# Attention on one core: products with V and row sums in four 32-column tiles instead of two 64-column tiles

## What is computed

```python
def _attn_ref(q, k, v, centroids):
    ...
    mask = q_assign[:, :, :, None] == k_assign[:, :, None, :]
    scores = scale * np.matmul(q, k.transpose(0, 1, 3, 2))
    scores = np.where(mask, scores, -1000000000.0)
    scores = scores - np.max(scores, axis=-1, keepdims=True)
    attn = np.exp(scores)
    attn = attn / (np.sum(attn, axis=-1, keepdims=True) + 1e-09)
    return np.matmul(attn, v).astype(np.float32)

def reference(**kwargs):
    attn_out = _attn_ref(**attn_kwargs)
    x = np.ascontiguousarray(attn_out.transpose(0, 2, 1, 3)).reshape(B * S, H * D)
    x = _moe_ref(x=x, **moe_kwargs)
    return _moe2_ref(x=x, **moe2_kwargs)
```

## Time and profile before

| what | value |
|---|---|
| median of 3 runs | 753.73 us (753.08 to 753.86) |
| the profiled execution's own time | 754.39 us |
| span of the profile, first to last instruction | 752.6 us |
| TensorE matmul busy | 730.7 us, 97% |
| VectorE, ScalarE, GpSimd busy | 504.8, 425.9, 362.3 us |
| mean granted TensorE clock | 0.991 of full speed |
| one step of the attention part | 13.9 us |

### The profile page before, as it was taken

One profiled execution on the slowest core, in us unless ns is written; L12 is line 12 of the kernel. 1 busy time (PEld: TensorE's weight loads), 2 busy tenths in 40 slices (PEclk: granted clock), 3 DMA queues, 4 the chain that ended last, 5 costly groups with the idle time before them and its releaser, 6 DMA issues.

```text
span 752.6 us, 10229 instructions
## 1 busy us (share of the span) xinstructions
PE 730.7 (97%) x3633; PEld 571.0 (76%) x3633; DVE 504.8 (67%) x796; ACT 425.9 (57%) x734; POOL 362.3 (48%) x271
## 2 busy tenths in 40 slices
PE   4799999999999999999999999999999999999998
PEld 2556656656657588888888888878779999998886
DVE  6888888888864486768777686774975555643211
ACT  4366766666755788878676777773442333223221
POOL 4058688688685646652222223541636466551000
PEclk9699999999999999999999999999999999999999
DMA  7336565454331442000000032003100011000111
GB/s 153 69 92 157 135 158 136 107 126 108 91 77 32 134 133 78 1 0 1 1 0 2 1 111 75 39 0 113 57 28 29 29 30 30 27 1 14 57 43 56
DMA packets 62002, 47.59 MB, mean 63 GB/s; under 512 B 29856, under 2 KB 54272, under 8 KB 61952
## 3 DMA queue, kind: packets, MB, share of 16 engines
q1 hardware_dynamic: 61952, 46.94, 23.0%
HBM read 28.35 MB, written 3.15 MB: 42 GB/s over the span
## 4 chain that ended last, share of the span: by engine, by line
PE 93%; DVE 3%; ACT 2%; issue 1%; DMA 1%; POOL 0%; SPq 0%; DVEq 0%; ACTq 0%
PE psum L1127 91%; PE psum L1132 2%; DVE psum L1638 1%; PE psum L661 1%; DMA RAWQK<-in_k 1%; DVE YS L864 1%; DVE OPS L1573 1%; ACT P L1421 0%; DVE MROW L1638 0%; DVE WT L677 0%; DVE YS L858 0%; ACT WC L754 0%; ACT OPS L1397 0%; PE psum L1205 0%; ACT OPS L1385 0%
## 5 line engine op out<-in xcount | busy, mean ns | idle before, releaser
L1127 PEld LDWEIGHTS psum<-OPS 128*128 128x128 f32 x576 | 98.5, 193 | 52.7 <-issue 38.0
L1127 PE MATMUL psum<-OPS 128*128 128x384 f32 x576 | 130.0, 362 | 6.7 <-DVE psum L1638 2.6
L539 POOL TENSOR_TENSOR G<-TT,G 128x512 fp32r<-128x512 f32 x48 | 62.3, 1299 | 152.0 <-ACT G L424 152.0
L1799 POOL TENSOR_TENSOR PSUMS<-PSUMS,P 128x768 f32<-128x768 f32 x64 | 107.9, 1686 | 18.6 <-ACT P L1421 12.2
L1421 ACT ACTIVATE P<-psum 128x768 f32<-128x768 f32 x96 | 76.2, 808 | 48.0 <-PE psum L1127 46.7
L1638 DVE TENSOR_REDUCE psum<-psum 128x1 f32<-128x768 f32 x90 | 86.2, 958 | 24.0 <-PE psum L1127 23.9
L1127 PE MATMUL psum<-G,WSPLIT 128*128 128x512 f32 x360 | 86.6, 390 | 1.1 <-POOL G L539 1.1
L1127 PE MATMUL psum<-XT,WSPLIT 128*128 128x512 f32 x360 | 86.5, 389 | 0.0
L469 DVE SCALAR_TENSOR_TENSOR HH<-UU,ABSB,psum 128x512 f32<-128x512 f32 x48 | 35.9, 748 | 67.6 <-ACT TT L402 67.6
L1127 PEld LDWEIGHTS psum<-G,WSPLIT 128*128 128x128 f32 x360 | 67.4, 188 | 15.5 <-POOL G L539 1.5
L1127 PEld LDWEIGHTS psum<-XT,WSPLIT 128*128 128x128 f32 x360 | 67.6, 188 | 14.0
(11 more groups left out here) (126 smaller groups left out, 1240.6 us busy)
## 6 DMA issues: line engine op xcount, KB each, us to landing
OPS<-OPS SPq DMA_DIRECT2D x32, 192.0 KB, 3.0
W3R<-in_moe_w SPq DMA_DIRECT2D x8, 512.0 KB, 3.4
RAWF<-in_moe_w SPq DMA_DIRECT2D x16, 256.0 KB, 3.1
RAWQK<-in_q SPq DMA_DIRECT2D x16, 192.0 KB, 3.1
RAWQK<-in_k SPq DMA_DIRECT2D x16, 192.0 KB, 3.7
V<-in_v SPq DMA_DIRECT2D x16, 192.0 KB, 2.9
XT<-XH SPq DMA_DIRECT2D x32, 96.0 KB, 2.2
XT<-XL SPq DMA_DIRECT2D x32, 96.0 KB, 2.2
```

What stands on the lines that cost most here:

```text
L539: nc.gpsimd.tensor_tensor(G[:, n % 2, 1, :], TT[:, n % 4, :], G[:, n % 2, 0, :].bitcast(F32), ALU.subtract).then_inc(g_lo, 1)
L1127: return nc.tensor.matmul(o, stationary, moving, start=start, stop=stop, skip_group_check=True)
L1799: nc.gpsimd.tensor_tensor(total, P32[:, (2 * u) % 4, :, 0:HALF] if n == 1 else total, P32[:, (2 * u + n) % 4, :, 0:HALF], ALU.add).then_in ...
```

## The change

The queries are cut into four quarters of 192 rather than two halves of 384, and V's 64 columns into the even and the odd ones (h = 0, 1). A product with V becomes eight: for each h and each quarter g a stationary operand 128 by 32 (every second column of V) and 194 moving columns, the result in partitions 32g to 32g+31, columns h*194 on. The row sums become four products with 32 columns of ones and 192 moving columns. Output row 32g+r, half h, is then column 2r+h of the head's output for quarter g. SUMS and LB are 192 columns wide; VOUT and X32 keep their 384 columns in two halves h, and `take_out` needs one operation for each half since VMEAN differs. x is placed by eight transfers of 64 rows by 192 columns.

```diff
-            P32 = ph("P32", [P, 4, 2, HALF + 2], F32)
+            P32 = ph("P32", [P, 4, 4, QS + TAIL], F32)
...
-            LB = ph("LB", [P, HALF], F32)
-            VOUT = ph("VOUT", [P, HALF], F32)
-            VMEAN = ph("VMEAN", [P, 1], F32)
+            LB = ph("LB", [P, QS], F32)
+            VOUT = ph("VOUT", [P, 2, QS], F32)
+            VMEAN = ph("VMEAN", [P, 2], F32)
...
-        SUMS = psum[:, 7, 0:HALF]
+        VO_MEAN = psum[:, 6, 0:2 * (QS + TAIL)].rearrange("p (h n) -> p h n", h=2)
+        SUMS = psum[:, 7, 0:QS]
...
-        X_COPIES = 4 * 16
+        X_COPIES = 8 * 16
...
-                    for x in range(2):
-                        sp.dma_start(XT[to, e, x_cols(u) + x * HALF:x_cols(u) + (x + 1) * HALF].bitcast(F32),
-                                     src[x * D:x * D + D, u % 2].bitcast(F32)).then_inc(x_placed[u % 2], 16)
+                    for g in range(4):
+                        sp.dma_start(XT[to, e, x_cols(u) + g * QS:x_cols(u) + (g + 1) * QS].bitcast(F32),
+                                     src[g * QUAD:(g + 1) * QUAD, u % 2].bitcast(F32)).then_inc(x_placed[u % 2], 16)
...
-                for x in range(2):
-                    last = mm(SUMS[x * D:(x + 1) * D], ONES, PSUMS[:, u % 2, x * HALF:(x + 1) * HALF], True, True)
+                for g in range(4):
+                    last = mm(SUMS[g * QUAD:(g + 1) * QUAD], ONES, PSUMS[:, u % 2, g * QS:(g + 1) * QS], True, True)
...
-                for x in range(2):
-                    last = mm(VO_MEAN[x * D:(x + 1) * D], V[:, u % 2, n, :], P32[:, (2 * u + n) % 4, x, :], n == 0, n == NT - 1)
+                for h in range(2):
+                    for g in range(4):
+                        last = mm(VO_MEAN[g * QUAD:(g + 1) * QUAD, h], V[:, u % 2, n, h::2], P32[:, (2 * u + n) % 4, g, :],
+                                  n == 0 and h == 0, n == NT - 1)
...
-                nc.scalar.activation(P32[:, (2 * u + n) % 4, :, 0:HALF], score_banks(u, n), ACT.Exp,
+                nc.scalar.activation(P32[:, (2 * u + n) % 4, :, 0:QS].rearrange("p (x y) n -> p x y n", x=2),
+                                     score_banks(u, n).rearrange("p x (y n) -> p x y n", y=2), ACT.Exp,
...
-                nc.scalar.copy(VMEAN, VO_MEAN[:, HALF:HALF + 1]).then_inc(v_mean, 1)
+                nc.scalar.copy(VMEAN, VO_MEAN[:, :, QS]).then_inc(v_mean, 1)
                 act.wait_ge(v_mean, u + 1)
-                nc.scalar.activation(VOUT, VO, ACT.Identity, bias=VMEAN).then_inc(v_out, 1)
+                for h in range(2):
+                    last = nc.scalar.activation(VOUT[:, h], VO_MEAN[:, h, 0:QS], ACT.Identity, bias=VMEAN[:, h:h + 1])
+                last.then_inc(v_out, 1)
...
-                nc.vector.scalar_tensor_tensor(X32, VOUT, -1.0, SUMS, ALU.mult, ALU.mult).then_inc(x_made, 1)
+                nc.vector.scalar_tensor_tensor(X32, VOUT, -1.0, SUMS.rearrange("p (o n) -> p o n", o=1).broadcast_to([P, 2, QS]),
+                                               ALU.mult, ALU.mult).then_inc(x_made, 1)
```

More of the change, by code:

```diff
@@ L43, in build @@
     HALF = S // 2
+    QS = S // 4
+    TAIL = 2
     KT = DM // P
@@ L86, in build @@
             OPS = ph("OPS", [P, 4, 4, S], F32R)
-            P32 = ph("P32", [P, 4, 2, HALF + 2], F32)
+            P32 = ph("P32", [P, 4, 4, QS + TAIL], F32)
             V = ph("V", [P, 2, NT, D], F32)
-            ONES = ph("ONES", [P, D], F32)
+            ONES = ph("ONES", [P, QUAD], F32)
             PSUMS = ph("PSUMS", [P, 2, S], F32)
-            X32 = ph("X32", [P, HALF], F32)
-            XH = ph("XH", [P, 2, HALF], F32R)
-            XL = ph("XL", [P, 2, HALF], F32R)
-            LB = ph("LB", [P, HALF], F32)
-            VOUT = ph("VOUT", [P, HALF], F32)
-            VMEAN = ph("VMEAN", [P, 1], F32)
+            X32 = ph("X32", [P, 2, QS], F32)
+            XH = ph("XH", [P, 2, 2, QS], F32R)
+            XL = ph("XL", [P, 2, 2, QS], F32R)
+            LB = ph("LB", [P, QS], F32)
+            VOUT = ph("VOUT", [P, 2, QS], F32)
+            VMEAN = ph("VMEAN", [P, 2], F32)
             NM = ph("NM", [P, 8], F32)
-            ph("GAP_P", [P, 39], F32)
+            ph("GAP_P", [P, 39 + 207], F32)
             ph("GAP_HH", [P, 5 * CH], F32)
@@ L160, in build @@
         VO = psum[:, 6, 0:HALF]
-        VO_MEAN = psum[:, 6, 0:HALF + 2]
-        SUMS = psum[:, 7, 0:HALF]
+        VO_MEAN = psum[:, 6, 0:2 * (QS + TAIL)].rearrange("p (h n) -> p h n", h=2)
+        SUMS = psum[:, 7, 0:QS]
         SIM = psum[:, 7, 0:HALF]
@@ L1556, in _ @@
             nc.vector.memset(ONES, 1.0)
-            nc.vector.memset(P32[:, :, :, HALF:HALF + 2], EMPTY_SUM / S).then_inc(consts_set, 1)
+            nc.vector.memset(P32[:, :, :, QS:QS + TAIL], EMPTY_SUM / S).then_inc(consts_set, 1)
             dve.wait_ge(act_chain, 3)
@@ L1797, in add_probs @@
                     pool.wait_ge(p_added, (NT - 1) * u + n - 1)
-                total = PSUMS[:, u % 2, :].rearrange("p (h n) -> p h n", h=2)
-                nc.gpsimd.tensor_tensor(total, P32[:, (2 * u) % 4, :, 0:HALF] if n == 1 else total,
-                                        P32[:, (2 * u + n) % 4, :, 0:HALF], ALU.add).then_inc(p_added, 1)
+                total = PSUMS[:, u % 2, :].rearrange("p (h n) -> p h n", h=4)
+                nc.gpsimd.tensor_tensor(total, P32[:, (2 * u) % 4, :, 0:QS] if n == 1 else total,
+                                        P32[:, (2 * u + n) % 4, :, 0:QS], ALU.add).then_inc(p_added, 1)
             def x_lo(u):
```

## The result

The changed kernel is slower, by half a per cent: 757.51 us (median of 14 runs, 754.99 to 761.93) against 753.86 us (14 runs, 753.08 to 754.87). The ratio is 1.0051, with a 95% interval from 1.0036 to 1.0065. The forecast was 749.8 us, in a range up to 753.3.

A forecast was written before the change was run, and what follows sets the result against it. TensorE was taken to bound the kernel, busy all of its 13.90 us step. Step 1 -0.46, steps 2 to 5 0, 6 to 12 -2.2, 13 -0.32, last sums -0.97: -4.0 us, giving 749.8 us, range 746.8 to 753.3.

The forecast's parts named there:

- TensorE's part: TensorE's attention steps: shorter row sums and one tile-shape change less save 6.8 us together; a step goes from 13.92 to 13.46.
- The rate of issue: Rival, 7%: in the 96 steps with V TensorE can't issue small pairs fast enough; at 52 ns a pair, 764 us.
- ScalarE's hand-over: After the products with V: VOUT 0.74 for 0.58 us, Ln and Exp 0.16 less each; up to 0.07 us lost a step.
- Short rows of 192: Exponents and GpSimd's adds in shorter rows: taken at nothing, bounds 0 and 0.05 us for each exponent; with non-overlapping tiles a 7% rival.
- What SyncE takes back: SyncE's queue: four more issues, 2.56 us, delay the maxima; a step gains 0.32 us, not 0.46, and steps 2 to 5 nothing.
- The rival on SyncE: 14%: SyncE holds TensorE more, +0.5 us in each of steps 2 to 5, gain 0.12 in seven steps: 753.1 us.
- The first rival: 22%: SyncE doesn't hold TensorE; the full -6.8 us less ScalarE's 0.07 in 13 steps: 747.3 us, at best 746.9.

The follow-up runs named there:

- e1: The changed kernel with both parts of x side by side in one buffer, so four transfers of x a unit instead of eight: 746.32 us, ratio 0.9904.
- e9: The kernel before with its layouts and four x transfers, only TensorE's products with V and row sums cut into four tiles: 752.04 us, ratio 0.998.
- e11: e1 with ScalarE's reciprocals moved behind the second exponent and VectorE's first division behind the maxima: 747.79 us, ratio 0.9927.
- e2: The kernel before with each transfer of x cut in two, eight a unit, nothing else changed: 757.6 us, ratio 1.0051.
- e10: e9 with x in eight transfers, cut as in e2: 761.03 us, ratio 1.0091.
- e5: e2 with 25 more TensorE instructions ahead of each product with V, asking for a semaphore long reached: 964.68 us, ratio 1.2792.

## Why the prediction was wrong, point by point

- **TensorE's part: right.** 0.79, 1.78 and 1.44 us in place of 0.80, 1.78 and 1.44; with SyncE out of the way (e1) the step is 13.44 us for a forecast of 13.46 and the kernel 7.5 us faster, for a forecast of 6.8. No run accounts for the other 0.7 us.
- **The rate of issue: right.** The groups above leave no room for a slower pair: a product with V alone takes 0.79 us, and less 0.14 for the change of tile shape that is 0.65 us for sixteen pairs, 41 ns each. e9 shows the same with unchanged layouts. The Trainium skill (TensorE: Matmul & The Clock Gate, section "Wait — 56ns, not 53.3ns?") has about 62 ns for each matmul with hardware decoding off. This case's trace shows no such bound; no row tells how instructions are decoded here.
- **ScalarE's hand-over: right in size, and no bound.** The two VOUT operations take 0.73 us together, forecast 0.74, and Ln and Exp 0.16 less each, in ScalarE's timeline of the change:

```profile
165.30 0.73 ACT L1437 ACTIVATE VOUT<-psum,VMEAN 128x192 f32<-128x192 f32 x2
165.93 0.42 ACT L1443 ACTIVATE LB<-psum,EPS 128x192 f32<-128x192 f32 x1
166.38 0.37 ACT L1445 ACTIVATE LB<-LB 128x192 f32<-128x192 f32 x1
```

What was expected to stay behind of TensorE's gain, up to 0.07 us a step, can't be seen: e1's step is no longer than TensorE's own sum, and e11, which takes these operations out of the way, wins nothing.

- **Short rows of 192: right at nothing.** An exponent takes 810 ns, it took 808; an add on GpSimd 1690, it took 1686.
- **"What SyncE takes back": the step that failed.** Its mechanism was right: four more issues, the maxima late, TensorE waiting for them, steps 2 to 5 without room. Its size was not, and the term that failed is the long issues. The list's terms (7.04, 2.56, 0.64, 0.8 and 4 x 0.64) add up to 13.6 us, not to the 13.8 written, and 13.6 is what a list without a long issue takes (e2). The forecast left steps 2 to 5 at their 13.9 us, which has 0.3 us a step for long issues, and the rival gave them 0.5 more. They come about once a step with the longer program, and steps 2 to 5 take 14.91 us: 1.3 us more than the list, and 1.0 more than the 13.9 of before, that is +4.0 us where the sum has 0. In steps 6 to 11 the masks go out every 13.95 us ((204.10 - 120.40) / 6), not every 13.6: the same long issues fall ahead of the maxima there. From step 6 to 13 that is +0.5 us where the sum has -2.2. Where they hardly come in, the forecast held: between 162.27 and 189.50, with one group of issues 0.45 us too long, TensorE's two steps take 27.23 us for a forecast of 27.13.
- **What was not counted at all:** that 1216 more products make TensorE's program longer, and that fetching it meets SyncE's issues. Between e2 and e10 the longer program costs 14.96 - 14.30 = 0.66 us a step, and 3.4 us of the whole. Without it (that is, at e2's price) the change would have come out near 757.5 - 3.4 = 754.1, about level with before, an estimate. Even that is outside the range I gave, so the long issues that come with the shorter program too, of which the earlier trace rows shows one, were priced too low as well: e2's steps 2 to 5 take 14.30 us.
- **The rival on SyncE** had the right direction and stopped at 753.1 us, since it allowed 0.5 us a step, half of what these steps lost. The first rival, that SyncE doesn't hold TensorE, has a slip in its sum: 753.7 - 6.8 + 13 x 0.07 is 747.8, not 747.3.

What is shown: four issues for each unit are worth 11.2 us in this kernel (e1), 9.0 with the old layouts (e9 and e10) and 3.8 with the shorter program (e2). That the longer program makes SyncE's list slower is shown by e2 against e10, though TensorE's step is a little shorter in e10 and what else runs beside an issue may shift with it. That the fetches are the link is argued from their meeting in time and from the counts; the run that was to add fetches alone (e5) slowed TensorE too much to tell. How a fetch delays an issue stays open.

## What to carry to other kernels

When one engine is busy all the time and a change shortens its step, add up the whole list of issues of every queue for a step, with those that take long, and compare it with the new step: SyncE's list of steps 2 to 5 was 11.0 us without its long issues (13.6 - 4 x 0.64) in a step of 13.9, and 13.6 against TensorE's 13.5 afterwards, and then all that had been hidden in it counted. Pay for transfers by their number: laying two results side by side in one buffer, so that one transfer carries both, turned this change from +3.7 to -7.5 us. Work moved to another place in a full list only moves the wait to the next item, so look at what stands behind the new place as well.

## What the runs showed of the hardware

- An issue on SyncE takes 0.63 to 0.68 us whether it moves 48 or 96 KB (four took 2.52 and 2.70 us), but some take 1.1 to 1.9 us, and in the change every one that is over 0.3 us late meets a fetch of program code of 0.9 to 1.5 us. Kernels with some 2,500 more instructions have 38 fetches in place of 29.
- Small products are cheap: pairs of load and product in four tiles of 32 columns run at 41 ns each, and changing the tile shape around a group costs 0.14 us (a product with V and the similarities behind it take 1.44 us in place of 1.58 with the change between them gone).
- A semaphore that has long been reached isn't free to ask on TensorE: the kernel got 0.089 us slower for each of 2400 added instructions, of which about 0.06 us is the ask, an estimate, and the rest goes with the lower granted clock.
